# Low pieces of the normalised rows moved behind the rotations, new first and last steps, and keys loaded ahead of the query copies

## The reference

```python
q_rot, k_rot = rotate(q), rotate(k)            # 4 x 8 heads, 576 tokens, 64 features; halves turned by cos and sin
scores = scale * q_rot @ k_rot.T
attn = exp(scores - rowmax); attn /= attn.sum + 1e-9
x = (attn @ v), laid out as 2304 tokens x 512
x = (sigmoid(x @ w_gate) * (x @ w_val)) @ w_out          # 512 -> 1536 -> 512
h = x @ w_in                                             # 512 -> 1024
solu = h * softmax(h); ln = (solu - mean) / sqrt(var + 1e-6) * g_ln
out = ln @ w_out2                                        # 1024 -> 512
```

## Time and profile before

| what | us |
|---|---|
| median of 3 runs (lowest, highest) | 920.6 (917.0, 924.54) |
| the profiled execution | 920.06 |
| its span, first to last instruction | 918.3 |
| busy: TensorE / VectorE / ScalarE / GpSimd | 891.1 / 433.0 / 340.4 / 385.0 |
| attention steps 2 to 13 (start of Q to start of Q) | 44.0 to 219.7 |
| granted clock, mean of the span | 0.995 |

### The profile page before, as it was taken

How to read it: one execution, slowest core, us unless ns; L and a number is a source line. 1 busy time by engine, 2 the same in 40 slices (tenths; PEclk the granted TensorE clock), 3 DMA queues, 4 the chain that set the end, 5 groups by cost and what they waited for, 6 DMA issues and landing times.

```text
span 918.3 us, 17061 instructions
## 1 busy us (share of the span) xinstructions
PE 891.1 (97%) x6272; PEld 711.0 (77%) x6272; DVE 433.0 (47%) x771; ACT 340.4 (37%) x743; POOL 385.0 (42%) x246
## 2 busy tenths in 40 slices
PE   8799999999899999999999999999999999999998
PEld 6466666666678898888888888888888888888886
DVE  5577777777723333242432243234434654444441
ACT  4688888888721111111111111111111443333332
POOL 4689999888347041023006006004757322222200
PEclk9999999999999999999999999999999999999999
DMA  8356566564421002002002001001110000000001
GB/s 266 89 168 197 155 189 181 175 195 127 127 82 59 10 1 70 0 1 69 1 1 70 1 0 35 10 0 32 59 46 1 1 35 17 18 23 23 23 23 47
DMA packets 35253, 60.33 MB, mean 66 GB/s; under 512 B 8464, under 2 KB 18192, under 8 KB 35216
## 3 DMA queue, kind: packets, MB, share of 16 engines
q1 hardware_dynamic: 33776, 59.00, 21.0%
q10 hardware_dynamic: 1440, 0.82, 0.3%
HBM read 44.80 MB, written 5.37 MB: 55 GB/s over the span
## 4 chain that ended last, share of the span: by engine, by line
PE 77%; POOL 15%; issue 6%; DMA 1%; DVE 1%; SPq 1%; ACT 0%; POOLq 0%; DVEq 0%; ACTq 0%
PE ps L1218 32%; PE ps L1252 16%; PE ps L1318 11%; PE ps L1290 11%; POOL raw_k L667 4%; POOL q_lo L688 2%; POOL raw_q L667 2%; POOL rot_q L672 2%; POOL k_lo L688 2%; POOL x_lo L708 2%; PE ps L1150 2%; PE ps L1199 2%; PE ps L1302 1%; PE ps L1111 1%; PE ps L1178 1%
## 5 line engine op out<-in xcount | busy, mean ns | idle before, releaser
L1218 PE MATMUL ps<-x_hi,w_hi 128*128 128x512 f32 (+1 forms) x480 | 177.0, 369 | 0.0
L1218 PE MATMUL ps<-x_lo,w_hi 128*128 128x512 f32 (+1 forms) x480 | 176.7, 368 | 0.0
L1218 PE MATMUL ps<-x_hi,w_lo 128*128 128x512 f32 (+1 forms) x480 | 176.6, 368 | 0.0
L1039 DVE TENSOR_TENSOR hid<-ps,sig 128x512 f32<-128x512 f32 (+1 forms) x60 | 38.3, 638 | 241.6 <-PE ps L1218 210.0
L873 ACT ACTIVATE sig<-ps 128x512 f32<-128x512 f32 (+1 forms) x60 | 33.3, 555 | 304.6 <-PE ps L1218 304.6
L736 POOL TENSOR_SCALAR w_hi<-raw_w 128x1024 fp32r<-128x1024 f32 x15 | 41.3, 2775 | 215.5 <-PE ps L1252 215.4
L956 DVE TENSOR_REDUCE nmax<-ps 128x1 f32<-128x576 f32 x144 | 108.6, 755 | 38.5 <-PE ps L1150 37.7
L1218 PEld LDWEIGHTS ps<-x_hi,w_hi 128*128 128x128 f32 x480 | 90.5, 189 | 15.7 <-issue 0.9
L833 ACT ACTIVATE prob<-ps,nmax 128x576 f32<-128x576 f32 x128 | 94.8, 741 | 20.9 <-DVE nmax L956 14.9
L1218 PEld LDWEIGHTS ps<-x_hi,w_lo 128*128 128x128 f32 x480 | 90.5, 189 | 15.2
L1218 PEld LDWEIGHTS ps<-x_lo,w_hi 128*128 128x128 f32 x480 | 90.5, 189 | 14.7
(11 more groups left out here) (115 smaller groups left out, 1623.3 us busy)
## 6 DMA issues: line engine op xcount, KB each, us to landing
raw_q<-in_q SPq DMA_DIRECT2D x15, 640.0 KB, 5.0
raw_k<-in_k SPq DMA_DIRECT2D x15, 640.0 KB, 4.4
q_hi<-q_hi SPq DMA_DIRECT2D x28, 160.0 KB, 2.7
q_lo<-q_lo SPq DMA_DIRECT2D x28, 160.0 KB, 2.8
out_y<-y_sb SPq DMA_DIRECT2D x17, 256.0 KB, 2.0
v_sb<-in_v SPq DMA_DIRECT2D x16, 256.0 KB, 2.6
rrep<-inverses SPq DMA_DIRECT2D x16, 256.0 KB, 3.4
raw_w<-in_moe_w_gate SPq DMA_DIRECT2D x6, 512.0 KB, 3.5
```

What stands on the lines that cost most here:

```text
L1218: last = nc.tensor.matmul(in_parts(gv_ps[f][n][:, 0:size(c)], c), w, x, start=m == 0, stop=m == len(todo) - 1)
```

## The change

All of it lies in the attention steps and around them.

1. XL leaves the steps. VectorE writes the float32 rows of a pair to `x_rows`, which has the addresses of `x_lo`, and no longer waits for the x_lo of the pair before. GpSimd makes all x_lo in place behind its rotations (`rests`): pairs 0 to 7, then the low pieces of two weights, pairs 8 to 14, the third weight, pair 15.
2. SyncE: LK ahead of T; T also holds until the first score tile of the current pair is made. The copies of pair 1 count on a semaphore of their own.
3. Step 0: turns AB1 and AB0 one score tile later, with ScalarE's copies of them; other numbers of fillers. Step 1: ScalarE makes qh first and kh behind S1, which had been behind S3 and S6.
4. Step 15: the casts of the first two weights behind the maxima of S5 and S6 instead of S3 and S4. Step 16: the third cast behind AB3y, and the first quarter of the gate product between Q and K instead of behind AB3.

```diff
--- before.py
+++ after.py
@@ -117,6 +117,10 @@
         alloc(ends, "x_lo_first", [P, PAIRS * S - QN])
         tab_q = alloc(ends, "tab_q", [P, 2, QM + TAIL])
         ends.close()
+        rows = ExitStack()
+        alloc(rows, "x_hi_all", [P, PAIRS * S])
+        x_rows = alloc(rows, "x_rows", [P, PAIRS * S])
+        rows.close()
         x_hi = alloc(ctx, "x_hi", [P, PAIRS * S], F32R)
         x_lo = alloc(ctx, "x_lo", [P, PAIRS * S], F32R)
 
@@ -151,7 +155,6 @@
         rinv = alloc(at, "rinv", [P, 2, NARROW])
         rinv_t = alloc(at, "rinv_t", [SLOTS, P])
         rrep = alloc(at, "rrep", [P, S])
-        x_f = alloc(at, "x_f", [P, S])
         at.close()
 
 
@@ -219,7 +222,7 @@
         q_rot, k_rot = sem("q_rot"), sem("k_rot")
         q_hi, k_hi = sem("q_hi"), sem("k_hi")
         q_lo, k_lo = sem("q_lo"), sem("k_lo")
-        q_twice = sem("q_twice")
+        q_twice, q1_twice = sem("q_twice"), sem("q1_twice")
         pe_holds, sp_holds = sem("pe_holds"), sem("sp_holds")
         turned_inverses = sem("turned_inverses")
         zeros_ready = sem("zeros_ready")
@@ -290,22 +293,22 @@
         ORDER_PE = ["Q", "S0", "S1", "K", "AB2", "S2", "PV0a", "S3", "AB3", "S4", "PV0b", "S5", "AB1", "S6", "PV0", "AB0", "S7", "S8", "PV1"]
         ORDER_ACT = ["qh", "Qx", "Qy", "S0", "Ky", "S1", "AB2x", "S2", "AB3x", "S3", "S4", "AB1x", "S5", "S6", "AB0x", "kh", "S7", "S8", "AB1y"]
         ORDER_DVE = ["S0", "Kx", "S1", "S2", "AB2y", "S3", "S4", "AB3y", "S5", "S6", "PV0", "S7", "S8", "AB0y", "INV", "PV1"]
-        ORDER_POOL = ["ql", "RQ", "kl", "RK", "XL"]
-        ORDER_SP = ["LQ", "RW", "RR", "LV", "T", "LK"]
-        FIRST_PE = ["S0", "S1", "S2", "S3", "S4", "S5", "AB1", "S6", "AB0", "S7", "S8"]
-        FIRST_ACT = ["S0", "qB", "S1", "S2", "S3", "S4", "S5", "AB1x", "S6", "AB0x", "S7", "S8", "AB1y"]
+        ORDER_POOL = ["ql", "RQ", "kl", "RK"]
+        ORDER_SP = ["LQ", "RW", "RR", "LV", "LK", "T"]
+        FIRST_PE = ["S0", "S1", "S2", "S3", "S4", "S5", "S6", "AB1", "S7", "AB0", "S8"]
+        FIRST_ACT = ["S0", "qB", "S1", "S2", "S3", "S4", "S5", "S6", "AB1x", "S7", "AB0x", "S8", "AB1y"]
         FIRST_DVE = ["S0", "kB", "qB", "S1", "S2", "S3", "S4", "S5", "S6", "S7", "S8", "AB0y", "INV"]
         FIRST_SP = ["LV", "T"]
         SECOND_PE = ["Q", "S0", "S1", "K", "AB2", "S2", "PV0a", "S3", "AB3", "S4", "PV0b", "S5", "S6", "AB1", "PV0", "S7", "AB0", "S8", "PV1"]
-        SECOND_ACT = ["Qx", "Qy", "S0", "Ky", "S1", "AB2x", "S2", "AB3x", "S3", "qh", "S4", "S5", "S6", "kh", "AB1x", "S7", "AB0x", "S8", "AB1y"]
-        SECOND_POOL = ["ql", "kl", "RQ", "XL", "RK"]
+        SECOND_ACT = ["qh", "Qx", "Qy", "S0", "Ky", "S1", "kh", "AB2x", "S2", "AB3x", "S3", "S4", "S5", "S6", "AB1x", "S7", "AB0x", "S8", "AB1y"]
+        SECOND_POOL = ["ql", "kl", "RQ", "RK"]
         LAST_PE = ["Q", "K", "AB2", "AB3", "PV0a", "PV0b", "PV0", "PV1"]
         LAST_ACT = ["Qx", "Qy", "Ky", "AB2x", "AB3x"]
         LAST_DVE = ["Kx", "AB2y", "AB3y", "PV0", "PV1"]
         WARM = 17
-        FILL = {"S1": 5, "S2": 12, "S3": 1, "S4": 1, "S5": 1, "S6": 1, "S7": 1}
-        BETWEEN = {"AB3": (0,), "PV0": (1, 2), "PV1": (3,)}
-        AHEAD = {"AB2": -1, "AB3": -1, "K": -1, "Q": -1, "PV0a": -1, "PV0b": -1, "PV0": -1, "PV1": -1, "XL": -1, "RW": -1, "RR": -1, "qh": 1, "kh": 1, "ql": 1, "kl": 1, "T": 1, "RQ": 2, "RK": 2, "LK": 2, "LQ": 2}
+        FILL = {"S1": 5, "S2": 6, "S3": 1, "S4": 2, "S5": 1, "S6": 4, "S7": 1, "S8": 6}
+        BETWEEN = {"Q": (0,), "PV0": (1, 2), "PV1": (3,)}
+        AHEAD = {"AB2": -1, "AB3": -1, "K": -1, "Q": -1, "PV0a": -1, "PV0b": -1, "PV0": -1, "PV1": -1, "RW": -1, "RR": -1, "qh": 1, "kh": 1, "ql": 1, "kl": 1, "T": 1, "RQ": 2, "RK": 2, "LK": 2, "LQ": 2}
         ITEMS = [n for n in ORDER_PE if n[:2] == "AB" or n in ("K", "Q")]
         RING = [(n, r) for n in ITEMS for r in range(2)]
         BANK = {n: i % 3 for i, n in enumerate(RING)}
@@ -522,16 +525,18 @@
 
             def twice_q(p):
 
-                pieces = q_pieces[par(p)]
+                pieces, done = q_pieces[par(p)], q_twice
                 if early(p, 2):
                     sp.wait_ge(q_rot, 1)
-                    pieces = [q_plain[1]]
+                    pieces, done = [q_plain[1]], q1_twice
                 else:
+                    if not early(p, 3):
+                        hold(sc_full, num(p) * SLOTS - SLOTS + 1)
                     sp.wait_ge(q_lo, num(p) - 1)
                 for x in pieces:
                     for r in range(2):
                         sp.dma_start(x[ROWS[r], SIDE:SIDE + WIDE].bitcast(F32), x[ROWS[1 - r], 0:WIDE].bitcast(F32)
-                                     ).then_inc(q_twice, 16)
+                                     ).then_inc(done, 16)
 
             def twice_first(r, cols):
 
@@ -696,18 +701,12 @@
                     rest(p, [x[:] for x in k_pieces[par(p)]], rot_k[:], k_hi, k_lo)
                 elif name == "ql" and not head_first(p):
                     rest(p, [x[:, 0:WIDE] for x in q_pieces[par(p)]], rot_q[:], q_hi, q_lo)
-                elif name == "XL":
-                    if step == PAIRS - 1:
-                        pool.wait_ge(sc_full, (PAIRS - 1) * SLOTS)
-                        lows(0, 0, (0, 1))
-                    if step == PAIRS:
-                        pool.wait_ge(sc_full, PAIRS * SLOTS)
-                        lows(0, 0, (2,))
-                    hold(x_norm[1], num(p) + 1)
-                    cols = bass.ds(num(p) * S, S)
-                    nc.gpsimd.tensor_tensor(x_lo[:, cols], x_f[:], x_hi[:, cols].bitcast(F32),
-                                            ALU.subtract).then_inc(x_ready, 1)
-
+
+            def rests(p):
+
+                cols = slice(p * S, p * S + S)
+                nc.gpsimd.tensor_tensor(x_lo[:, cols], x_rows[:, cols], x_hi[:, cols].bitcast(F32),
+                                        ALU.subtract).then_inc(x_ready, 1)
 
             for tab in tab_q_in:
                 pool.wait_ge(tab, 16)
@@ -726,6 +725,19 @@
             pool.wait_ge(k_prod, 1)
             nc.gpsimd.tensor_tensor(k_plain[1][:, extra], raw_k[:, 0, extra], raw_k[:, 1, extra], ALU.add).then_inc(k_rot, 1)
             pipeline(pool, ORDER_POOL, item, second=SECOND_POOL)
+            pool.wait_ge(x_norm[1], 2 * HP)
+            for p in range(2 * HP):
+                rests(p)
+            pool.wait_ge(sc_full, (PAIRS - 1) * SLOTS)
+            lows(0, 0, (0,))
+            lows(0, 0, (1,))
+            pool.wait_ge(x_norm[1], PAIRS - 1)
+            for p in range(2 * HP, PAIRS - 1):
+                rests(p)
+            pool.wait_ge(sc_full, PAIRS * SLOTS)
+            lows(0, 0, (2,))
+            hold(x_norm[1], PAIRS)
+            rests(PAIRS - 1)
 
 
             def weights(g, u):
@@ -988,16 +1000,14 @@
                     dve.wait_ge(rrep_in, num(p) * 16 + 16)
                 else:
                     dve.wait_ge(rrep_tails_in, num(p) * 32 + 32)
-                if n == 0 and not early(p, 1):
-                    dve.wait_ge(x_ready, num(p))
                 if early(p, 1):
                     dve.wait_ge(q_rot, 2)
                     dve.wait_ge(k_rot, 2)
                 if isinstance(p, int) and p >= PAIRS - 2:
                     dve.wait_ge(k_rot, PAIRS - 1)
                     dve.wait_ge(q_rot, PAIRS - 1)
-                nc.vector.tensor_tensor(x_f[:, a:b], o_ps[:, 0:b - a], rrep[:, a:b], ALU.mult).then_inc(x_full, 1)
                 cols = bass.ds(num(p) * S + a, b - a)
+                nc.vector.tensor_tensor(x_rows[:, cols], o_ps[:, 0:b - a], rrep[:, a:b], ALU.mult).then_inc(x_full, 1)
                 nc.vector.tensor_tensor(x_hi[:, cols], o_ps[:, 0:b - a], rrep[:, a:b], ALU.mult).then_inc(x_norm[n], 1)
 
             def item(name, p, step):
@@ -1013,13 +1023,13 @@
                     first_rows(raw_q0, [(0, tab_q[:, :, 0:QM]), (S - QM, tab_q[:, :, QM:])], q_plain[0], slice(QM, WIDE), q0_prod, q0_rot)
                 elif name[0] == "S":
                     maxs(int(name[1:]), p)
-                    if step == PAIRS - 1 and name in ("S3", "S4"):
-                        first_weights(int(name[1:]) - 3)
+                    if step == PAIRS - 1 and name in ("S5", "S6"):
+                        first_weights(int(name[1:]) - 5)
                 elif name == "INV":
                     inverse(p)
                 else:
                     turned(name, p, step)
-                if step == PAIRS and name == "AB2y":
+                if step == PAIRS and name == "AB3y":
                     first_weights(2)
                 if step == PAIRS and name == "PV0":
                     hidden(0, 0, 0)
@@ -1119,7 +1129,7 @@
                     pe.wait_ge(exp_done, num(p) * SLOTS + (j - 1))
                 if j == 0 and not early(p, 2):
                     pe.wait_ge(k_lo, num(p) - 1)
-                    pe.wait_ge(q_twice, num(p) * 64 - 32)
+                    pe.wait_ge(q_twice, num(p) * 64 - 64)
                 if early(p, 1):
```

(2 more changed lines are left out.)

## The result

The changed kernel is slower: 928.61 us (median of 7 runs, 923.79 to 932.86) against 920.6 (917.0 to 924.54). The ratio is 1.0093, 95% interval 1.0072 to 1.0114. The forecast was 918.0 in a range of 912.5 to 923. The profiled execution of the changed kernel took 923.79 us (span 922.0), the fastest of the seven, so its trace shows 3.7 us of the 8.0 that the median lost.

A forecast was written before the change was run, and what follows sets the result against it. GpSimd and TensorE were taken to run neck and neck, TensorE setting the pace from step 7. Terms -1.8 + 0.5 - 0.3 - 0.2 - 0.7 = -2.5 us took 920.06 to 917.6; forecast median 918.0, range 912.5 to 923.

The forecast's parts named there:

- Part 2: SyncE's queue in the attention steps: key load ahead of the query copies, priced at +0.5 us.
- rival (b): S0 of pairs 3 to 15: copies behind the keys make it late, costing 5.5 us, giving 923.0; chance 0.13.
- the bundle: Query copies and key load together in SyncE's queue, taken as 6.74 us, slowest 7.42, in the new order too.
- my upper end: Cost of the keys-first order if the copies come strictly last behind the keys: 1.0 us.
- A late S0 gives the next copies more time: Argument against rival (b), in the attention loop: a late first score leaves the following copies more time; no size given.
- part 1: x_lo out of the loop: steps 2 to 6 fall to 14.49 us each, 1.8 us gained, nothing from later loop steps.
- rival (a): GpSimd paced the whole loop: all twelve loop steps fall to 14.09 us, gaining 6.6, giving 913.2; chance 0.12.
- Part 3: Steps 0 and 1: Q some 2 us sooner, mostly given back through kh; 0.3 us gained, bounds -1 and +2.
- My sign against the step on the fillers: First steps: a granted clock below full after 31 us would prove the forecast's zero price for the moved fillers wrong.
- Part 4: Steps 15 and 16: later weight casts gain 0.2 us, a gate product quarter between Q and K gains 0.7 us.
- Rival (c): Nothing moves: step 1 swallows all, DMA landings slow steps 2 to 6, the gate product waits; 920.6, chance 0.12.

The follow-up runs named there:

- copies_first: Changed kernel with the key load back behind the query copies in SyncE's queue, the rest kept: 917.33 us, ratio 0.9963 to the kernel before.
- queries_later: Changed kernel with each step's query load moved behind the write of the inverses, keys still ahead of the copies: 922.39 us, ratio 1.0017.
- keys_between: Changed kernel with the q_hi copies ahead of the key load and the q_lo copies behind it: 929.27 us, ratio 1.0091.
- old_first_steps: Changed kernel with step 0's lists, ScalarE's list of step 1 and the fillers of the kernel before: 932.05 us, ratio 1.0145.
- The fillers: Changed kernel with five matmuls, results thrown away, ahead of S0 from pair 2 on: 932.47 us; the same on copies_first: 931.58 us.
- x_lo_alone: Kernel before with only x_lo moved out of the loop, plus the added hold and semaphore for the copies: 921.26 us, ratio 1.0003.
- new_first_alone: Kernel before with only the new step 0 lists, ScalarE's step 1 list and fillers, plus the added hold and semaphore: 919.75 us, ratio 0.9988.
- keys_first_alone: Kernel before with only keys ahead of the query copies in SyncE's queue, with the hold and the semaphore: 930.7 us, ratio 1.0113.
- after_again: The changed kernel run again without an edit, for a second profile: 927.9 us, ratio 1.0081.

## Why the prediction was wrong

**The step that failed is Part 2's "+0.5 us".** It measured +6.7 us in the profiled execution (steps 2 to 14) and +11.3 in the median, each against copies_first, which differs only in this order. It is rival (b), which had a chance of 0.13. Its arithmetic had the right deadline: the key load goes out 7.98 us after Q (forecast 7.91), S0 is due at 14.8 (14.87). What failed is the bundle. I took 6.74 us from the first issue to the last landing, with 7.42 as the slowest, from an order in which 640 KB of keys came last. (There were twelve such bundles; the one that I left out, copies issued at 53.99 and key product at 61.51, was the slowest at 7.52.) In the new order keys and copies took 7.6 to 8.7 us in the seven waiting steps, where the deadline allowed 7. Two reasons, both seen in runs: the copies cost more behind the keys than ahead of them (q_lo 2.8 to 4.6 us), and that remains without the query load (4.7 in queries_later); and the query load is issued 1.9 us after the q_lo copies begin to be (160.53 against 158.63) and was not in my bundle (without it 5.3 us of waits are left, and the median falls by 6.2). I had held the bytes constant and taken the time to be constant with them. "A late S0 gives the next copies more time" was right: there were seven waits, not thirteen. But it did not make them cheap. Against the kernel before the loop and step 14 lose only 4.9 us, because part 1 gained there; against copies_first they lose 6.7 (loop 179.94 to 173.94, step 14 14.79 to 14.08), nearly all of the 7.1 us of waits. Seven waits of 0.4 to 1.6 us instead of the rival's twelve of 0.46 come near its 5.5 us by luck.
The Trainium skill (DMA: Bandwidth & Descriptors, Queues, rings and completion order) says that descriptors of one queue are taken in ring order on each DMA engine, which I had given only the weight of my upper end, 1.0 us. keys_between agrees with it: the copies ahead of the keys landed in 2.6 us and those behind them in 5.1.

**And a term that I had not priced at all.** Rival (b)'s own time, 923.0, nearly is the profiled execution's 923.79. The median is 4.8 higher. That part comes with the clock: a third of the waits of 0.8 us and more were followed by 1.2 GHz, which made steps of 15.1 to 16.2 us into steps of 16.5 to 19.2. The profiled executions of the changed kernel and of old_first_steps have none of these falls, and the other five traces have one to three each. Two of them, at the mean of the ten, 1.8 us, would make 3.7 of the 4.8; that is an estimate, since the execution at the median was not profiled and falls in other steps count as well. The fillers show it from the other side: covered waits, no low clock in the loop, and a scatter of 2.2 us. What decides whether a wait is followed by a fall stays open. I had watched the clock only in step 1, for the fillers there, and the trace of before has no wait in the loop long enough to show a fall. What stays open is step 15's share: it took 18.81 in the second trace of the changed kernel and 14.47 in the first, and the traces do not say why the first cast was held for two x_lo there.

**The rest held.** copies_first is the change without part 2; for it the same sum gives 920.6 - 3.0 = 917.6, and it measured 917.33. By its profile against that of before: loop -1.76 us (forecast -1.8), step 15 -0.15 (-0.2), from Q of step 16 on -0.81 (-0.7), first steps -0.07 (-0.3). These are single executions, and the first steps differ between them by more than their term. Point by point:
- Part 1: loop steps of 14.42 to 14.63 in copies_first, not 14.09; rival (a) is out. GpSimd waits for k_hi as forecast (changed kernel):

```profile
160.46 1.55 POOL L693 TENSOR_TENSOR k_lo<-rot_k,k_hi 128x640 fp32r<-128x640 f32 x1 [2.35 <-ACT k_hi L833]
```

 Alone, it moved the median by nothing (x_lo_alone, 921.26): the stall of step 2 is still there, and in the profiled execution the clock fell behind it; the runs without that loss show the 919 forecast.
- Part 3: Q of step 1 came 1.84 us sooner (24.02; in copies_first, with the same first steps, it came at 26.37), and k_hi and the AB2x copy stood where the sum had them (31.0; the changed kernel's ScalarE):

```profile
30.39 0.74 ACT L833 ACTIVATE k_hi<-rot_k 128x640 fp32r<-128x640 f32 x1 [0.84 <-POOL rot_k L677]
31.03 0.58 ACT L856 ACTIVATE pT<-ps 128x512 f32<-128x512 f32 x1
```

 so 0.25 us were left by Q of step 2 (0.07 in copies_first, -0.32 in new_first_alone). A gain of 0.3 is not shown: old_first_steps, with the old lists, has this Q at 42.83, sooner than any. My sign against the step on the fillers, a granted clock below full after 31 us, came true: the clock is 1.00 from 18.5 to 29.5 (0.69 before) and 0.84 from 29.5 to 40. In copies_first, with the same fillers, the slow stretch lies before 22 us, so a single trace does not tell where the fillers put it. Neither shows a price by Q of step 2.
- Part 4: K stands at once behind the gate product, and GpSimd was in time by what I had worked out: the first w_lo is ready at 248.71 + 2.82 = 251.5 and wanted at 254.03, 2.5 us later (forecast 2.6). GpSimd, then TensorE:

```profile
237.29 11.46 POOL L708 TENSOR_TENSOR x_lo<-x_rows,x_hi 128x576 fp32r<-128x576 f32 x8
248.71 2.82 POOL L665 TENSOR_TENSOR w_lo<-raw_w,w_hi 128x1024 fp32r<-128x1024 f32 x1
```

```profile
253.46 0.50 PE L1228 MATMUL ps<-x_hi,w_hi 128*128 128x512 f32 x1
...
254.03 0.40 PE L1228 MATMUL ps<-x_hi,w_lo 128*128 128x512 f32 x1
...
256.41 0.46 PE L1188 MATMUL ps<-eye_f,prob 64*128 64x64 f32 x8
```

 The eight x_lo took 11.46, as worked out (11.3). Rival (c) is out: with the keys behind the copies the changed kernel beats the one before by an interval that ends below 1 (0.995 to 0.9976), and parts 1 and 4 gained what they were to gain.

## What to carry to other kernels

When a small transfer that something waits for is moved behind a large one, don't carry over the time of the bundle: take the margin at the deadline, and count every transfer that is issued until the small one has landed, the next stage's loads too. Move the large one to where it has landed before the small one goes out, or leave it behind. And price an idle stretch of TensorE of 2 us by its own length and by the low clock that can follow it, which cost 1.1 to 2.6 us here where it did.

## What the runs showed of the hardware

- The granted clock falls inside a loop that is otherwise busy, and not by the length of the wait alone: three of three waits for q_lo above 1.8 us were followed by 1.2 GHz, 7 of 30 between 0.8 and 1.8, none of 15 below. A wait of 0.98 with one of 0.67 close behind was followed by a fall in x_lo_alone and keys_first_alone; 0.97 with 0.67 was not in old_first_steps.
- VectorE's cast of 128x1024 float32, 0.70 us with GpSimd idle, took 0.79 to 2.48 us beside GpSimd's subtractions. In the rows looked at, a cast that began while one of them ran ended 0.54 to 0.56 us after its end, or after the end of the next one. Either engine can pay. In the changed kernel's first trace the first cast took 0.82 and the x_lo behind it 1.87 instead of 1.41; in after_again the x_lo behind went first at its usual 1.45 and the cast took 2.25. A second cast that began behind the start of w_lo took 2.47 to 2.48 in three of three traces, and w_lo its usual 2.4. I had weighed this contention for GpSimd's side alone, by VectorE instructions with two SBUF inputs. The Trainium skill (GPSIMD Engine Reference, Key points) also names VectorE instructions in a 2-port mode as contending; no view here shows a cast's mode, but the rows agree that the two contend. On ScalarE the cast took 1.06 us in all four cases.
- Which of the two goes first when a cast comes while an x_lo runs (the cast in one execution, the next x_lo in another) is not explained.
